# Attention, MLP and experts in one kernel: half of the key transposes put ahead of the odd scores, one table load behind the key copies, and another order of the first pair's roots

## The reference

```python
mag = np.sqrt(a_re * a_re + a_im * a_im)
scale = np.minimum(mag, 0.999) / (mag + 1e-06)
a_re_n, a_im_n = (a_re * scale, a_im * scale)
for t in range(S):
    new_re = ar * S_re - ai * S_im
    new_im = ar * S_im + ai * S_re
    kv = np.einsum('bhd,bhe->bhde', k[:, :, t], v[:, :, t])
    S_re, S_im = (new_re + kv, new_im)
    y[:, :, t] = np.einsum('bhd,bhde->bhe', q[:, :, t], S_re)
...
out = (x @ w_a) * (x @ w_b) @ w_out
...
# each token to one of 8 experts: relu(x @ w1[e]) @ w2[e], times the gate
```

## Time and profile before

| | us |
|---|---|
| median of 3 runs | 1523.94 |
| lowest, highest | 1522.74, 1531.78 |
| time of the profiled execution | 1528.5 |
| its span, first to last instruction | 1526.8 |
| attention, start to the last output copy | about 623 |
| first work of the MLP on PE | about 641 |

### The profile page before, as it was taken

One profiled execution on the slowest core, in us unless ns is written; L12 is line 12 of the kernel. 1 busy time (PEld: TensorE's weight loads), 2 busy tenths in 40 slices (PEclk: granted clock), 3 DMA queues, 4 the chain that ended last, 5 costly groups with the idle time before them and its releaser, 6 DMA issues.

```text
span 1526.8 us, 32668 instructions
## 1 busy us (share of the span) xinstructions
PE 1297.7 (85%) x12942; PEld 1235.2 (81%) x12943; DVE 678.2 (44%) x1083; ACT 630.8 (41%) x1199; POOL 270.7 (18%) x193
## 2 busy tenths in 40 slices
PE   1798888888888887399999999999992399999998
PEld 1687777777787776299999999999991399999998
DVE  2679999989999984511111111111113112222121
ACT  5556666666666541422222222222222134444342
POOL 0000000000000000012121121211224355554541
PEclk9558898888989885599999999999995699999999
DMA  5112232222222214620000000000003433333220
GB/s 103 32 33 49 57 67 52 56 56 49 48 49 51 40 45 173 199 69 17 17 0 15 0 15 15 0 15 0 0 0 132 179 116 117 116 118 103 94 84 28
DMA packets 178703, 91.95 MB, mean 60 GB/s; under 512 B 153884, under 2 KB 169027, under 8 KB 178608
## 3 DMA queue, kind: packets, MB, share of 16 engines
q1 hardware_dynamic: 168880, 55.95, 15.6%
q0 software_dynamic: 9728, 34.64, 6.2%
HBM read 68.47 MB, written 23.66 MB: 60 GB/s over the span
## 4 chain that ended last, share of the span: by engine, by line
issue 33%; PE 13%; POOL 11%; ACT 1%; DMA 0%; POOLq 0%; ACTq 0%; DVEq 0%; SPq 0%; DVE 0%
PE e_h L1265 5%; PE e_y L1274 4%; POOL pl L959 4%; POOL w1l L962 3%; POOL w2l L963 3%; PE m_x L1165 1%; PE m_b L1155 1%; PE m_a L1155 1%; POOL out L1002 1%; PE e_tr L1244 0%; ACT ys L935 0%; DMA xe<-xs_scratch 0%; ACT w1h L884 0%; DMA out<-ys,idx 0%; POOLq L958 0%
## 5 line engine op out<-in xcount | busy, mean ns | idle before, releaser
L625 PE MATMUL score<-QT,KT 96*64 96x32 f32 x5376 | 206.9, 237 | 50.6 <-DVE KT L484 20.2
L625 PEld LDWEIGHTS score<-QT,KT 96*64 96x64 f32 x5376 | 194.6, 155 | 66.1 <-DVE KT L484 27.3
L1049 DVE TENSOR_TENSOR pr<-asb,m_b 128x384 f32<-128x384 f32 x96 | 53.2, 554 | 380.4 <-ACT asb L865 380.4
L959 POOL TENSOR_TENSOR pl<-pr,ph 128x384 fp32r<-128x384 f32 x96 | 96.4, 1008 | 417.4 <-ACT ph L869 417.4
L865 ACT COPY asb<-m_a 128x384 f32<-128x384 f32 x96 | 46.0, 479 | 277.1 <-PE m_b L1155 277.1
L1135 DVE SCALAR_TENSOR_TENSOR hl<-e_h,hh 128x256 fp32r<-128x256 f32 x128 | 52.8, 423 | 234.1 <-ACT hh L923 218.0
L1265 PE MATMUL e_h<-xeh,w1h 128*128 128x256 f32 x384 | 111.8, 291 | 22.3 <-issue 17.8
L1265 PE MATMUL e_h<-xeh,w1l 128*128 128x256 f32 x384 | 111.1, 289 | 0.0
L1265 PE MATMUL e_h<-xel,w1h 128*128 128x256 f32 x384 | 111.0, 289 | 0.0
L949 POOL MEMSET pads<- 128x385 f32 x1 | 0.4, 421 | 623.0 <-POOLq L111 623.0
L1155 PE MATMUL m_a<-xh,WH 128*128 128x384 f32 x288 | 102.1, 355 | 1.2 <-DVE xl L1033 1.2
(11 more groups left out here) (182 smaller groups left out, 3140.5 us busy)
## 6 DMA issues: line engine op xcount, KB each, us to landing
raw<-w POOLq DMA_DIRECT2D x16, 1536.0 KB, 9.1
xs_scratch<-pads SPq DMA_DIRECT2D x1, 7720.0 KB, 27.2
xe<-xs_scratch SPq DMA_DIRECT2D x17, 386.0 KB, 3.2
xin<-x_scratch SPq DMA_DIRECT2D x9, 576.0 KB, 3.9
raw_re<-a_re SPq DMA_DIRECT2D x32, 144.0 KB, 2.9
raw_im<-a_im SPq DMA_DIRECT2D x32, 144.0 KB, 3.2
raw_k<-k SPq DMA_DIRECT2D x32, 144.0 KB, 3.0
raw_q<-q SPq DMA_DIRECT2D x32, 144.0 KB, 3.4
```

The lines of the kernel that those rows point to most:

```text
L625: last = pe.matmul(score[n % 2][CH * g:CH * g + CH, a * HALF:(a + 1) * HALF], KT[i][0:R2, h, c * CH:(c + 1) * CH], x, start=True, stop=True)
L959: pool.tensor_tensor(pl[:, f % 4, :], pr[:, f % 2, :], ph[:, f % 4, :].bitcast(F32), ALU.subtract).then_inc(s["pl_done"], 1)
L1049: dve.tensor_tensor(pr[:, f % 2, :], asb[:, f % 2, :], bp_[f % 2][:, 0:TW], ALU.mult).then_inc(s["prod_done"], 1)
```

## The change

Five edits, all in `attention`:

- PE: groups 0 and 1 of the key transposes of unit t - 1, with the wait for its last update, stand ahead of `scores(t, 1)`; groups 2 and 3 stay behind it.
- ACT: the load of `trig_and_small` stands behind the four key copies and right ahead of the arctangent.
- ACT: the load of `natural_log_exp_and_others` is asked for ahead of everything, and the one ahead of the first roots is left out.
- ACT: `roots(0)` comes ahead of `squares(1)`.
- DVE: the wait for the constants moves from ahead of all stages to stage 0.

```diff
@@ scalar @@
+            act.preload_act_table_set("natural_log_exp_and_others")
             act.wait_ge(s["bias_set"], 1)
             squares(0)
             for t in STAGES:
-                if live(t + 1):
-                    act.preload_act_table_set("trig_and_small")
                 if live(t - 1):
                     for f in range(4):
                         keys_out(t - 1, f)
                 if live(t + 1):
+                    act.preload_act_table_set("trig_and_small")
                     angle(t + 1)
                     repeat_decay(t + 1)
...
-                if live(t + 3):
+                if live(t + 3) and t + 3 != 1:
                     squares(t + 3)
...
                 if live(t + 2):
-                    act.preload_act_table_set("natural_log_exp_and_others")
+                    if t + 2:
+                        act.preload_act_table_set("natural_log_exp_and_others")
                     roots(t + 2)
+                if t + 3 == 1:
+                    squares(1)
@@ vector @@
-            dve.wait_ge(s["const_in"], 32)
             for t in STAGES:
                 L, A2, A1, Y = live(t), live(t + 1), live(t + 2), live(t - 1)
+                if t == 0:
+                    dve.wait_ge(s["const_in"], 32)
@@ tensor @@
+                if Y:
+                    pe.wait_ge(s["updated"], update_no(t - 1, UPDATES))
+                    for f in both:
+                        keys(t - 1, f)
                 if L:
                     pe.wait_ge(s["updated"], update_no(t, 1))
                     scores(t, 1)
                 if Y:
-                    pe.wait_ge(s["updated"], update_no(t - 1, UPDATES))
-                    for f in range(4):
+                    for f in (2, 3):
                         keys(t - 1, f)
                     increments(t - 1)
```

## The result

The changed kernel takes 1564.99 us (median of 4 runs, 1564.76 to 1568.49) against 1526.31 for the kernel before beside it. The ratio is 1.0256 (95% interval 1.0218 to 1.0293). I had forecast 1497 with a range of 1488 to 1507.

The account below looks back on a forecast made before the run. DVE, waiting for score product 2 behind PE's key transposes and increments, was taken as the bound. Move 18.0, start 5.2 and clock 3.4 made 26.6 us off the median 1523.9: about 1497, range 1488 to 1507.

Parts of the forecast that it names:

- The bound: DVE has the most work, 31.69 us a middle stage; it waits almost only for product 2, 26.1 us in stages 2 to 14.
- The move: Two groups of key transposes ahead of product 1 make increments and product 2 earlier: 18.0 us less, clock left as is.
- The clock: PE denser where its clock falls: at least nothing, at most 10.3 us more gained; a third taken, 3.4 us.
- The rival of the other side: PE's clock rises later behind transposes, increments and product 2: 1.9 us longer in 13 stages, 1544 us, chance 0.03.
- The table load: ACT's load between last key copy and arctangent: counted 0, with 0.1 or 0.2 us lost at worst in stage 7.
- The start: First logarithm near 9.0 us, 5.6 earlier, and unit 0's chain with it: counted 5.2 us, bounds 3.6 and 5.6.
- The two rules of the Trainium skill: On ACT, a table load adds a 1.38 us drain; on PE, transposes don't raise the clock: prediction's trace against both.

Follow-up runs that it names:

- move_only: The kernel before with only groups 0 and 1 of the key transposes moved ahead of product 1: 1594.83 us, ratio 1.0444.
- table_only: The kernel before with only the arctangent's table load moved behind the key copies: 1526.28 us, ratio 1.0005.
- after_fill_all: The changed kernel with 2, 3, 4 and 6 extra matmuls ahead of product 1, the increments, product 2 and product 3: 1482.15 us, ratio 0.9716.
- fill_1_3: The kernel before with five extra matmuls ahead of product 1 and six ahead of product 3: 1489.38 us, ratio 0.9764.
- fill_1_3_start: The kernel before with five extra matmuls ahead of product 1, six ahead of product 3, and the three start edits: 1492.46 us, ratio 0.9777.
- balanced: The changed kernel with the second half of the increments moved from ahead of product 2 to behind the turned decays: 1513.12 us, ratio 0.9911.
- balanced_q: The changed kernel with only the last quarter of the increments moved from ahead of product 2 to behind the turned decays: 1552.92 us, ratio 1.0177.

## Why the prediction was wrong, point by point

**The bound.** Right: DVE's 31.7 us are the floor of a stage, and its wait for product 2 was what could be won. The kernels with full clock stand at 32.09. Not right was that the part behind the attention runs at full clock throughout: the earlier trace rows has 5, 5 and 6 among its last 24 slices.

**The move.** The local numbers came out in the stage shown. Idle ahead of product 1: 0.39 us (0.3 or less forecast). Increments 2.8 us behind product 1's start: 2.78. DVE's first wait at the merge: gone. Wrong was the step "every microsecond that the increments start earlier is a microsecond off the stage", from which the 18.0 us came. I followed DVE to the end of its wait and did not ask what PE does next. PE is then early as well; it turns the decays and stands idle until DVE's update, and before the change this gap was 0.8 us, since the increments had come late. The time was not won but passed on, from DVE ahead of L501 to PE ahead of product 3 (1.31 us now).

**The clock.** This is the step that turned the sign. I had it as "at least nothing: the falls stay", with a gain of 3.4 us. The sum took it that the slow stretch doesn't move with the work. It did: it began 0 to 3 us into a stage before, and now there are two, some 3.7 and 13.7 us into it. The change had put idle time right ahead of the phases, a long piece of PE with DVE behind it: 3.3 us a stage. By the sum, stages 2 to 14 were to be (15.8 + 3.4) / 13 = 1.5 us shorter on average than their 34.2, and were 3.4 longer. Over the two profiled executions that makes 43.9 us. The first key update comes 6.1 earlier, stages 0 and 1 are 0.2 longer together, the end of the attention takes 3.4 less up to the MLP's first work, and the MLP and the experts, where nothing was changed, 5.3 more: 40.0 in all, the whole difference of their spans.

**The rival of the other side.** "PE stays at half clock longer" was there, with a chance of 0.03 and 1544 us. Its price, 20 us, was half of the loss, and its mechanism was another: I looked for a late rise behind the increments, and what came was a second fall behind them. move_only came nearer to what I had described, 27 us without a rise. The argument against it (the increments stay together) looked at one piece only. A chance of 0.03 was far too little for a kernel in which the clock goes up and down in every stage.

**The table load.** Right as "0" in the time (table_only), but not as "0.1 or 0.2 us lost at worst": the long stages lose 1.2 us at the arctangent and have it back at product 2. Together with the move it is worth 25 us, which I had not seen: without it ACT's load keeps the banks of groups 2 and 3.

**The start.** The chain did move by 5.8 us (8.79 against 14.61; 5.6 forecast). In the time it doesn't show (0.9987, interval 0.9961 to 1.0014): the kernel before itself spreads over 1517 to 1534 us, and the first stages run more or less of their length at half clock. table_only, which has the start of the kernel before, shows how much that can be: its stages 0 and 1 took 33.44 and 34.89 us in the profiled execution, against 42.06 and 36.03 before. So such swings are larger than the 5.2 us of the start. That the gain is lost in them is likely, and not shown.

**The two rules of the Trainium skill.** The Trainium skill, "ScalarE: Activation LUTs", section "What ACT_TABLE_LOAD costs", adds a drain of 1.38 us to a load. In the changed kernel the arctangent starts 1.30 us behind the start of the load (276.06 against 274.76), so there was none to be seen. For the transposes, see above.

**Open.** Whether the move is worth anything once the clock stays up. In the middle stages it is not: they take 32.09 us with it (after_fill_all) and without it (fill_1_3), near DVE's own 31.6, and the first key update of stage 16 comes at 533.61 with it and at 533.14 without it (fill_1_3_start). At the two ends it can't be told: 1482 against 1482 to 1499, and the two differ in fillers as well. Why balanced settles into the rhythm without a gap ahead of product 3, and balanced_q into the one with it, was seen and not explained; nor was it why the clock, once down, comes back after 3 us in one place and after 27 in another.

## What to carry to other kernels

Where the trace shows TensorE's clock falling in every round of a loop, first ask of a change where it will leave TensorE idle, on which engine's account the removed wait turns up again, and what runs right behind that gap; a shorter chain can be dearer than a longer one. Cheap matmuls into unused columns of a bank, in two to four gaps where TensorE waits for another engine, held the clock and gave 2.4 to 2.8% here. One gap alone was not enough: filled ahead of product 1 or of product 3, it only moved the fall. Measure the parts of a change together and apart: here move and table load were 4.4% slower and 0.0% apart, 2.9% together.

## What the runs showed of the hardware

The profiles of kernels with the same instructions have PE busy for 28.9 to 37.8 us in a stage, by the clock alone: a score product takes 1.59 us at 1.00 and 2.78 at 0.50, half of the increments (ten records) 1.09 and 1.91, the phases 3.6 and 6.9. PE can be busy for 27 us on end at half clock, with short matmuls and transposes, and not be given the full one (move_only, 26.81 of 27.30 us). And the stages settle into lengths that repeat to 0.04 us: 37.55 in the changed kernel, 34.14 in balanced, and with the move alone 41.02 with one of 33.9 after every few.
